# Attention tiles woven with a gated feed-forward layer: where PE's transposes, one output chunk and one gate product stand in the order

## The reference, cut to what matters

```python
scores = scale * np.matmul(q, k.transpose(0, 1, 3, 2))
kth = np.partition(scores, -32, axis=-1)[..., -32:-31]
scores = np.where(scores >= kth, scores, -1e9)
attn = exp(scores - max); attn /= sum + 1e-9
x = matmul(attn, v)                      # 1152 rows x 512
xn = x / sqrt(mean(x * x) + 1e-6) * rms_g
g = xn @ w_gate                          # 512 -> 1536
x = (g / (1 + exp(-g)) * (xn @ w_val)) @ w_out
e = argmax(x @ gate)                     # then 512 -> 1024 -> 512 by expert e
```

## Time and profile before

| | us |
|---|---|
| median of 3 runs (lowest, highest) | 656.95 (656.74, 657.01) |
| the profiled execution, its own time | 656.66 |
| its span (first to last instruction) | 654.7 |
| PE busy in the span | 618.9 (95%) |
| DVE busy | 411.6 (63%) |
| ACT busy | 327.0 (50%) |
| POOL busy | 264.0 (40%) |

### The profile page before, as it was taken

How to read it: one execution, slowest core, us unless ns; L and a number is a source line. 1 busy time by engine, 2 the same in 40 slices (tenths; PEclk the granted TensorE clock), 3 DMA queues, 4 the chain that set the end, 5 groups by cost and what they waited for, 6 DMA issues and landing times.

```text
span 654.7 us, 11169 instructions
## 1 busy us (share of the span) xinstructions
PE 618.9 (95%) x3954; PEld 476.5 (73%) x3954; DVE 411.6 (63%) x912; ACT 327.0 (50%) x713; POOL 264.0 (40%) x366
## 2 busy tenths in 40 slices
PE   7789799999999999999999999999999999999994
PEld 5466565775765765766766766756679999999994
DVE  4999997898897997997996996911111111111110
ACT  4777866756756766766766766753210101111100
POOL 1876774464364364454453553652310100111101
PEclk9799999999999999999999999999999999999998
DMA  9899800000000000000000000000396866767501
GB/s 241 203 367 354 207 2 0 18 18 2 17 18 1 18 17 1 18 17 2 18 17 2 2 17 1 1 18 1 122 389 208 273 224 246 252 215 266 170 2 38
DMA packets 55182, 65.45 MB, mean 100 GB/s; under 512 B 32282, under 2 KB 32282, under 8 KB 55132
## 3 DMA queue, kind: packets, MB, share of 16 engines
q1 hardware_dynamic: 53388, 60.05, 28.6%
q0 software_dynamic: 1744, 4.76, 2.0%
HBM read 52.89 MB, written 12.30 MB: 100 GB/s over the span
## 4 chain that ended last, share of the span: by engine, by line
PE 82%; ACT 8%; POOL 5%; issue 3%; POOLq 0%; ACTq 0%
PE ps L818 11%; PE ps L804 11%; PE ps L548 11%; PE ps L535 7%; PE ps L539 7%; PE ps L536 7%; PE ps L505 5%; PE ps L478 5%; PE ps L489 5%; PE ps L463 3%; POOL s_ring L1490 2%; ACT pt L877 2%; PE ps L563 2%; POOL hid L1427 2%; ACT z_pair L1012 1%
## 5 line engine op out<-in xcount | busy, mean ns | idle before, releaser
L1490 POOL TENSOR_TENSOR s_ring<-s_ring,z_pair 128x576 f32<-128x576 f32 x72 | 100.9, 1424 | 70.0 <-ACT z_pair L1012 70.0
L1307 DVE MATCH_REPLACE8 w_top<-m,w_top 128x576 f32<-128x576 f32 x144 | 105.8, 741 | 0.0
L1301 DVE MAX8 m<-w_top 128x8 f32<-128x576 f32 x144 | 101.5, 746 | 0.0
L548 PE MATMUL ps<-wo_space,hid 128*128 128x512 f32 x216 | 99.3, 593 | 0.4 <-issue 0.4
L535 PE MATMUL ps<-w_parts,x_hi 128*128 128x512 f32 x196 | 81.8, 417 | 0.0
L536 PE MATMUL ps<-w_parts,x_hi 128*128 128x512 f32 x196 | 77.4, 395 | 0.0
L818 PE MATMUL ps<-arena,w_loads 128*128 128x168 f32 x512 | 75.8, 307 | 0.5 <-issue 0.5
L804 PE MATMUL ps<-arena,w_loads 128*128 128x168 f32 x512 | 74.3, 306 | 0.6 <-ACT arena L877 0.6
L1513 POOL DMA_INDIRECT out_rows<-arena,s_ring x16 | 15.1, 942 | 147.0 <-DVE arena L1331 144.6
L804 PEld LDWEIGHTS ps<-arena,w_loads 128*128 128x128 f32 x512 | 73.3, 190 | 0.9 <-ACT arena L877 0.9
L818 PEld LDWEIGHTS ps<-arena,w_loads 128*128 128x128 f32 x512 | 73.2, 190 | 0.6 <-issue 0.6
(11 more groups left out here) (142 smaller groups left out, 903.9 us busy)
## 6 DMA issues: line engine op xcount, KB each, us to landing
w_loads<-in_moe_w SPq DMA_DIRECT2D x16, 2048.0 KB, 9.1
dispatched_rows<-drow SPq DMA_DIRECT2D x18, 260.0 KB, 8.0
w_loads<-in_moe_w_gate SPq DMA_DIRECT2D x3, 1024.0 KB, 7.6
w_loads<-in_moe_w_val SPq DMA_DIRECT2D x3, 1024.0 KB, 9.6
wo_space<-in_moe_w_out SPq DMA_DIRECT2D x1, 3072.0 KB, 11.6
arena<-dispatched_rows SPq DMA_DIRECT2D x8, 341.2 KB
out_rows<-drow SPq DMA_DIRECT2D x9, 256.0 KB, 5.1
q_space<-in_q SPq DMA_DIRECT2D x8, 256.0 KB, 3.0
```

Of the source, the lines that this page charges most:

```text
L548: last = mm(blk[0], hid[:, c * P:(c + 1) * P], wo_s[:, c, :], start=(c == 0), stop=(c == CF - 1))
L1301: vec.max(m8[:, 2 * (n % 2) + a, i, :], w_top[:, a, :]).then_inc(s["top_step"], 1)
L1307: vec.match_replace(w_top[:, a, :], m8[:, 2 * (n % 2) + a, i, :], w_top[:, a, :], NEG).then_inc(s["top_step"], 1)
L1490: gp.tensor_tensor(row, row, z_pair[:, a, :], ALU.subtract).then_inc(s["lowered"], 1)
```

## The change

PE: in the column slot (tiles after the first, while there is attention left) the transposes of half 0 stand between the eight high and the four low matmuls of G0. In the second slot (likewise) the transposes of half 1 and the rest stand between the high and the low matmuls of G1. In the output slot the chunks 6 to 9 are cut in two, and chunk 6 is multiplied ahead of the columns' turn. ACT: the copy of turned half 0 comes ahead of the score rows of half 1 in the column slot, and ahead of `q_columns` in the second slot; there the copies of half 1 and the rest come ahead of the tanh. POOL: the third gate product moves from the end of the third slot into the output slot, behind `far` and the bias and ahead of the subtraction of the marks.

```diff
-OUT = ((6, 0, 3), (7, 3, 6), (8, 6, 10), (9, 10, 11), (9, 11, 12))
+OUT = ((6, 0, 3), (7, 3, 6), (8, 6, 7), (8, 7, 10), (9, 10, 11), (9, 11, 12))
...
+            def gate_high(t, i):
+                pe.wait_ge(s["silu_done"], t * 3 + i)
+                block_high(t, wg_hi[:, :, i * 512:(i + 1) * 512], wg_lo[:, :, i * 512:(i + 1) * 512], blk[1])
+
+            def gate_low(t, i):
+                block_low(t, wg_hi[:, :, i * 512:(i + 1) * 512], blk[1])
...
-                    dense(n, BETA)
-                    if probs:
+                    if t > 0 and probs:
+                        gate_high(t, 0)
                         turn_probs(g, 0)
+                        gate_low(t, 0)
+                    else:
+                        dense(n, BETA)
+                        if probs:
+                            turn_probs(g, 0)
                     turn_out(n)
...
-                    if not early:
+                    around = due(n, BETA, G[1]) if probs and not early else None
+                    if around is not None:
+                        gate_high(around, 1)
+                    elif not early:
                         dense(n, BETA)
                     turn_out(n)
                     if probs:
                         turn_probs(g, 1)
                         turn_rest(g)
+                    if around is not None:
+                        gate_low(around, 1)
+                    t = due(n, GAMMA, OUT[2][0])
+                    if t is not None:
+                        ffn_out(t, 2)
                     turn_back_columns(n)
                     dense(n, GAMMA)
...
                         probs(g, 1)
+                    if here and t > 0:
+                        turned_probs(g, 0)
                     if n + 1 < NG:
                         score_rows(n + 1, 1)
-                    if here:
+                    if here and t == 0:
                         turned_probs(g, 0)
...
+                    around = here and n > FIRST + 1 and due(n, BETA, G[1]) is not None
+                    if around:
+                        turned_probs(g, 0)
                     if next_tile(n) is not None:
                         q_columns(next_tile(n))
-                    if here:
+                    if around:
+                        turned_probs(g, 1)
+                        turned_probs(g, 2)
+                    if here and not around:
                         turned_probs(g, 0)
                     dense(n, BETA)
                     out_turned(n)
-                    if here:
+                    if here and not around:
                         turned_probs(g, 1)
                         turned_probs(g, 2)
...
+                if due(n - 1, GAMMA, V[2]) is not None:
+                    gate_by_value(due(n - 1, GAMMA, V[2]), 2)
                 if t is not None and t > 0:
                     norm_last(t)
```

More of the change, by code:

```diff
@@ L530, in ffn_block, with block_high @@
                     return
+                block_high(t, w_hi, w_lo, bank)
+                block_low(t, w_hi, bank)
+            def block_high(t, w_hi, w_lo, bank):
                 pe.wait_ge(s["x_hi_set"], CD * t + CD - 1)
@@ L536, in ffn_block, with block_low @@
                     mm(bank, x_hi[:, c * P:(c + 1) * P], w_lo[:, c, :], start=False, stop=False)
+            def block_low(t, w_hi, bank):
                 pe.wait_ge(s["t_free"], use["xn", t] + 1)
@@ L618, in turn_last_pair @@
             def turn_last_pair(n, t):
-                for i in (3, 4):
+                for i in (4, 5):
                     before = due(n, ALPHA, OUT[i][0])
@@ L624, in turn_last_pair @@
                         ffn_out(before, i)
-                    if i == 3:
+                    if i == 4:
                         pe.wait_ge(s["o_copied"], HP * (t + 1))
@@ L649, in dense @@
                     turn_hidden(t, 1)
-                for i in range(3):
+                for i in (0, 1, 3):
                     t = due(n, at, OUT[i][0])
@@ L1420, in dense, with gate_by_value @@
                                      hi[:, half[0]:half[1] + 1, cols], ALU.subtract).then_inc(s["w_lo_set"], 1)
-                for i in range(FB):
+                for i in range(FB - 1):
                     t = due(n, at, V[i])
                     if t is not None:
[L1424 to L1427, removed]
+                        gate_by_value(t, i)
+            def gate_by_value(t, i):
+                hb = hid[:, i * 512:(i + 1) * 512]
+                pool.wait_ge(s["silu_done"], t * 3 + i + 1)
+                pool.wait_ge(s["val_copied"], t * 3 + i + 1)
+                gp.tensor_tensor(hb, xrow[:], hb, ALU.mult).then_inc(s["val_done"], 1)
             def scale_rows(t, h0, h1):
```

## The result

The changed kernel took 646.92 us in the median of five runs (646.81 to 647.17), the kernel before 656.74 in five runs beside it (656.03 to 657.01). The ratio is 0.9852, with a 95% interval of 0.9838 to 0.9866. The forecast was 647.0.

A forecast was written before the change was run, and what follows sets the result against it. PE was taken to set the pace, so only its waits could be won: 0.5 + 3.6 + 1.5 + 1.0 + 3.4 = 10.0 us off 656.66 gives 646.7, plus 0.29 for the median, 647.0; range 643.3 to 650.5.

The forecast's parts named there:

- Part 1: Column slot, half 0 turned inside G0: a 0.54 us wait goes, but only 0.07 us a tile is won, 0.5 in seven.
- what is late next: Column slot: the router's product, waiting for ACT's copy of the output's turn, starts 1.38 us behind that turn.
- the slow start: Column slot, router's product: a start after a wait loses 0.07 us more, eight matmuls taking 1.03 instead of 0.96.
- Part 2: Second slot, half 1 and rest inside G1: the wait ahead of `values` goes, 0.52 x 7 = 3.6 us.
- rival B: Second slot: half 1 waits inside G1 for ACT's copy of half 0, 0.41 us seven times, 649.9 us; chance 0.10.
- Part 3: Output slot, third gate product behind the clip distance: marks start earlier, 0.21 x 7 = 1.5 us, plus 1.0 in the last.
- The gain of the chain: Output slot: with `far` computed early, the chain from marks through POOL's subtraction to the exp comes 1.01 us earlier.
- Part 4: Output slot, chunk 6 ahead of the columns' turn: covers the wait for ACT's copy, 0.42 x 8 = 3.4 us.
- Part 5: The cuts themselves, transposes inside open blocks: taken as 0 extra, at most 1.2 us for 14 cuts.
- Rival D: DVE sets the pace: PE's removed waits reopen elsewhere and late score rows add 3.4 us, 660.3 us; chance 0.03.

## Why the prediction was right

**The sum.** Each term, as predicted, as its undoing showed in the periods, and in the medians:

| part | predicted us | from the periods | in the medians |
|---|---|---|---|
| 1 column slot | 0.5 (7 x 0.07) | 0.09 a tile | 0.50 |
| 2 second slot | 3.6 (7 x 0.52) | 0.53 in six tiles, 0.10 in the last | 3.24 |
| 3 product | 2.5 (7 x 0.21 and 1.0) | 0.21 a tile, and 0.98 once | 2.64 |
| 4 chunk | 3.4 (8 x 0.42) | 0.42 a tile | 3.54 |
| 5 cuts | 0 | 0.00 | |
| sum | 10.0 | | 9.9 |

The kernel gained 656.74 - 646.92 = 9.82 us. The mechanism of each term was right; that the forecast came within 0.08 us is in part luck. The gain was 0.18 short of the 10.0, and the kernel before ran 0.21 lower beside the changed one than in the three runs from which the forecast started (656.74 against 656.95).

**Part 1, the term that decided the number.** The step "what is late next" is confirmed: the product waits, 1.38 us behind the turn, for the copy that the profile names. Without that step the forecast would have been 643.7. The prediction took 0.07 for the slow start from lengths, whose ends are modelled. By starts, product to values, it is 0.95 (257.86 to 258.81) against 0.90 (258.06 to 258.96 with the column slot undone), so 0.05, and 262.25 - 262.11 - 0.05 = 0.09 is what the period showed.

The prediction's other estimate, worked out from the Trainium skill ("TensorE: Matmul & The Clock Gate", section on single matmul latency, and "ScalarE: Activation LUTs", section on what a table load costs), put the turn-to-product time at 1.16 us, 0.22 lower; part 1 would then be worth 0.29 us a tile (the prediction says 0.28). The trace has 1.38 here too, as in the tail row, so the measured row was the one to take. ACT's copy starts 0.63 behind the turn, takes 0.60 and ends 0.15 before the product starts. The copy's length agrees with the estimate's 613 ns; what the estimate lacks lies ahead of the copy and behind it.

**Part 2.** Wait and cover were right in six of seven tiles, with the margin given as 0.09 us and 0.08 in the trace. The prediction held all seven periods to be alike, and here they are not: in the last second slot PE has no queries to turn, and ACT's copy of half 0 has no query copy to overtake; rival B's wait came there, 0.37 us, and only about 0.1 of the 0.52 was won. That is why the part is worth 3.24 and not 3.6. ACT's order alone is a quarter of the part.

**Part 3.** The gain of the chain is 1.02 us (2.04 to 1.02 between copy and subtraction) where 1.01 was worked out.

**Part 4.** The wait was covered by a chunk of 0.86 us, and the later copy of the columns cost nothing.

**Part 5.** From the first start of half 0 and the low part to the start of the output's turn it takes 256.48 - 255.11 = 1.37 us, as it took 260.73 - 259.36 = 1.37 in the other order. In the second slot 268.50 - 267.02 = 1.48 us stand against 272.85 - 271.37 = 1.48, where 271.37 is the start of the low part. The cuts are free; the taken value was the lower bound.

**DVE.** Its idle time ahead of the low part was forecast to fall to 1.5 and is 1.28 to 1.53, with 1.89 in the first period. Rival D does not hold in the changed kernel: with 2.45 us more of DVE's work a tile it takes the same time. The claim behind it, that the 2.21 us of idle were all of the slack, put the slack too small: the gap between the low part's end and its use comes on top.

Everything behind the woven stage moved along whole, as said: from the last turn that ends a period to the end of the program it is 654.7 - 447.1 = 207.6 us before and 645.1 - 437.5 = 207.6 after.

## What to carry to other kernels

When a wait is removed, take the next instruction of the same engine that reads something copied by another, and measure its round trip from a place where nothing stands between; here the wait removed was 0.54 us a tile, and only 0.09 of it was won until the copy that the second instruction waits for came sooner too. Work for such gaps need not be new: a long accumulating block can be cut where a copy has to be covered, at no cost in time. And the slack of an engine that does not set the pace is not its idle time alone but that and the time until its result is read. Last, look at the first and the last of the repeated places by themselves: here the last second slot lacked one step and lost most of its gain.

## What was not expected of the hardware

A wait cost a little more than its length: eight small matmuls take 1.03 us behind one and 0.96 without (0.05 us by starts), even where the wait is only 0.10 us. And transposes into another bank inside an open accumulation of fp32r matmuls took no time beyond their own 0.11 us each (1.37 us for half 0 and the low part in either order, 1.48 with half 1 and rest).
